# A routed two-layer expert stage on one core: eight pairs of token tiles in place of three

## The chip, the cores and the metric

One core of a Trainium2 chip runs the whole program once. The metric is device time in microseconds (us); lower is better. The kernel before took a median of 958.46 us in 3 runs (958.34 to 959.61). Engines are named as in the profile: PE (TensorE), DVE (VectorE), ACT (ScalarE), POOL (GpSimd), SP (SyncE, which here only starts DMAs).

## The reference

```python
def reference(...):                      # cut to what matters
    attn = _attn_ref(q, k, v)            # [4, 8, 768, 64] recurrent attention with decay
    x = attn as rows                     # 3072 tokens x 512
    x = (max(h, 0) + alpha * min(h, 0)) @ w_out      where h = x @ w_in       # 512 -> 2048 -> 512
    logits = cosine(x, expert_emb) / tau             # 8 experts
    e = argmax(logits);  gate = softmax(logits)[e]
    out = gate * (max(x @ w1[e], 0) @ w2[e])         # 512 -> 1024 -> 512, one expert per token
```

Only the last line is the subject here: each token goes through the two matrices of its own expert. The routing depends on the data.

## The kernel before

Tokens come out of the attention and of the first two-layer stage in six chunks of 512. The router ranks the tokens of each chunk, and POOL scatters each row into a table in HBM that holds one region of `CAP` rows for each expert. The expert stage, from about 614 us on, walks that table in **tiles of 128 rows**. All matrix products are taken in three passes (high x high, low x high, high x low), so every operand is split into a high part (ACT, a cast) and a low part (DVE, a subtraction).

The weights of one expert are 4 MB, loaded as four **chunks** of 1 MB: chunks 0 and 1 are w1, chunks 2 and 3 are w2. A chunk goes from HBM into its own staging buffer `raw[m]` (there is one of each, four in all), ACT casts it into the weight buffer `W` (`split_expert` on ACT, L1516), DVE subtracts (`split_expert` on DVE, L1233). `W` has two slots that alternate. Each loading of an expert's weights is a **run**, numbered from 0. SP's `expert_weights(e, run)` issues the four loads in the order 0, 1, 2, 3; each waits until DVE has split the same chunk of the run before (`s_lo`), and since SP works in order, a later load waits for the earlier ones too.

The stage has two parts. First **three pairs**: two tiles of the same expert are taken together. `up_two(i, g)` (L841, four groups of 24 matmuls with 256 columns) makes the hidden values already transposed; `h_two_high` (ACT) and `h_two_low` (DVE) split them; `expert_down(t, ...)` (L879) makes the output of each tile. `x_transpose(i, tt)` (L711) turns the rows of a later tile (`tt` steps after tile `4 * i`) in the middle of an `expert_down`. The three pairs are chosen (`choose_pairs`) from the counts of the first five chunks of tokens, from whole groups of 256 rows, so that they can start before the last chunk is ranked.

Then **single tiles**, from tile `LEAD` = 6 on, in the order of the experts (`perm`: the fullest one first, then the others by number). A single tile is `up` (L819, 24 matmuls of 512 columns), `x_transpose` of the tile two further on, and `expert_down` with `h_transpose` (L856) of the next tile in its middle. Every expert gets at least one single tile (`ntile` is raised to 1). `T_NEXT` holds, for a tile that begins an expert, the number of the next expert. ACT's `tile(t)` does, in this order: `w1_part` (casts w1 chunks of the expert after that of tile t+1, if tile t+1 begins one), `relu_half(t+1)`, `x_hi_part(t+2)`, `load_rows` (of tile t+3), `w2_part` (casts w2 chunks of the expert after that of tile t), `h_hi_part(t+1)`, `y_part(t)`. DVE's `tile(t)` has the same parts in the same order, with `relu_half` ahead of `w1_part`. The engines run in order, so what stands behind a cast that waits for a chunk waits as well.

`pads` writes 128 rows of padding behind each expert's last row, eight DMAs from SP. `load_rows` brings 128 rows of the table; in the pairs it is issued from SP, in the single tiles from ACT's queue. POOL scatters each finished tile to `out` (L1739).

## Time and profile before

| | us |
|---|---|
| median of 3 runs | 958.46 |
| profiled execution, its own time | 958.03 |
| span of the profiled execution | 955.7 |
| around the span (958.03 - 955.7) | 2.3 |
| PE busy | 944.6 (99%) |
| DVE busy | 605.5 (63%) |
| ACT busy | 274.2 (29%) |
| POOL busy | 250.2 (26%) |
| granted TensorE clock, mean | 0.997 |

A row of the timeline gives the start, the duration, engine, source line, operation, output<-input, count, and in brackets how long the engine had been idle and what ended that. Instructions of one kind that follow each other are merged into one row. The landing time of a DMA is counted from its issue.

### The profile page before, as it was taken

The numbers are of one execution on the slowest core, as the hardware profiler recorded it, in microseconds if no ns is written. First come the engines' busy times: TensorE is split into PE (matmuls) and PEld (weight loads), VectorE is DVE, ScalarE is ACT, GpSimd is POOL, SyncE is SP. The second block draws the span as 40 slices with busy tenths as digits, with TensorE's granted clock in tenths as the row PEclk, the third lists the DMA queues.
The fourth block names the chain that finished last, engine by engine and source line by source line (L and its number), as shares of the span: only waits on it lengthen the run. The fifth ranks groups of instructions, "written<-read, shape, count | busy, mean of one in ns | idle before, by whom it ended". The sixth has DMA issues, their size and how long they took to land.

```text
span 955.7 us, 16603 instructions
## 1 busy us (share of the span) xinstructions
PE 944.6 (99%) x5542; PEld 795.1 (83%) x5543; DVE 605.5 (63%) x1111; ACT 274.2 (29%) x410; POOL 250.2 (26%) x192
## 2 busy tenths in 40 slices
PE   8999999999999999999999999999999999999996
PEld 7888888888888888888888888899888888888885
DVE  5555589647973698459865887787763742523541
ACT  4222121112111211112111222255655543423541
POOL 4443214241424143413432122441100100000001
PEclk9999999999999999999999999999999999999998
DMA  8431297023001400140002302187936461423311
GB/s 307 159 133 56 82 391 235 1 89 133 0 0 45 174 0 0 44 154 1 1 23 78 112 0 88 54 332 271 394 139 255 159 269 44 157 93 119 135 42 54
DMA packets 29142, 115.22 MB, mean 121 GB/s; under 512 B 4864, under 2 KB 5248, under 8 KB 22929
## 3 DMA queue, kind: packets, MB, share of 16 engines
q1 hardware_dynamic: 21584, 96.12, 27.6%
q0 software_dynamic: 4336, 12.61, 3.4%
q10 hardware_dynamic: 3168, 5.79, 2.0%
q8 instruction: 32, 0.52, 0.2%
q14 instruction: 22, 0.17, 0.1%
HBM read 101.88 MB, written 26.30 MB: 134 GB/s over the span
## 4 chain that ended last, share of the span: by engine, by line
PE 98%; DVE 0%; DMA 0%; issue 0%; POOLq 0%; ACT 0%; SPq 0%; DVEq 0%
PE bank L726 28%; PE bank L744 27%; PE bank L879 16%; PE bank L819 12%; PE bank L841 4%; PE bank L621 2%; PE bank L665 2%; PE bank L637 2%; PE bank L856 2%; PE bank L711 1%; PE bank L654 1%; DMA attention<-in_qk 0%; PE bank L690 0%; DVE en_all L970 0%; PE bank L684 0%; PE bank L698 0%
## 5 line engine op out<-in xcount | busy, mean ns | idle before, releaser
L726 PE MATMUL bank<-activations_split,weights_split 128*128 128x512 f32 x1152 | 277.8, 391 | 0.0
L744 PE MATMUL bank<-weights_split,activations_split 128*128 128x512 f32 x1152 | 276.0, 389 | 0.0
L744 PEld LDWEIGHTS bank<-weights_split,activations_split 128*128 128x128 f32 x1152 | 216.2, 188 | 44.8
L726 PEld LDWEIGHTS bank<-activations_split,weights_split 128*128 128x128 f32 x1152 | 215.1, 188 | 45.8 <-issue 1.1
L1681 POOL TENSOR_TENSOR activations_split<-scratch,activations_split 128x512 fp32r<-128x512 f32 x84 | 117.0, 1393 | 311.7 <-ACT activations_split L1436 304.4
L1436 ACT CAST activations_split<-scratch 128x512 fp32r<-128x512 f32 x96 | 59.8, 623 | 412.2 <-DVE scratch L1013 412.2
L879 PE MATMUL bank<-weights_split,activations_split 128*128 (+1 forms) x648 | 159.7, 397 | 0.0
L879 PEld LDWEIGHTS bank<-weights_split,activations_split 128*128 128x128 f32 x648 | 118.1, 188 | 22.6
L1072 DVE SCALAR_TENSOR_TENSOR attention<-rows,en_all 128x512 f32<-128x512 f32 x140 | 135.0, 1005 | 0.5 <-DMA en_all<-en_rows 0.5
L1008 DVE TENSOR_SCALAR scratch<-bank,alpha 128x512 f32<-128x512 f32 x96 | 71.7, 747 | 99.3 <-PE bank L726 98.6
L819 PE MATMUL bank<-weights_split,activations_split 128*128 x504 | 118.2, 390 | 0.1
L819 PEld LDWEIGHTS bank<-weights_split,activations_split 128*128 128x128 f32 x504 | 94.4, 188 | 19.9 <-issue 0.5
L1739 POOL DMA_INDIRECT out<-scratch,y_token x27 | 33.5, 1242 | 277.2 <-ACT scratch L1549 276.9
L1233 DVE TENSOR_TENSOR weights_split<-attention,weights_split 128x2048 f32 (+1 forms) x30 | 67.9, 2285 | 14.1 <-ACT weights_split L1516 13.9
L1226 DVE TENSOR_SCALAR en_all<-bank 128x512 f32<-128x512 f32 x21 | 14.5, 691 | 92.3 <-PE bank L819 92.3
L1013 DVE SCALAR_TENSOR_TENSOR scratch<-bank,scratch 128x512 f32<-128x512 f32 x96 | 66.4, 691 | 3.3
L1516 ACT CAST weights_split<-attention 128x2048 f32 (+1 forms) x30 | 56.7, 1906 | 11.4 <-issue 6.5
L1242 DVE TENSOR_TENSOR activations_split<-bank,activations_split 128x512 fp32r<-128x512 f32 x42 | 26.9, 683 | 25.1 <-ACT activations_split L1535 25.1
L1703 POOL DMA_INDIRECT expert_rows<-rows,slot_i x24 | 31.0, 1290 | 30.0 <-DVE slot_i L1172 25.0
L841 PE MATMUL bank<-activations_split,weights_split 128*128 128x256 f32 x288 | 36.4, 284 | 0.0
L841 PEld LDWEIGHTS bank<-activations_split,weights_split 128*128 128x128 f32 x288 | 35.3, 192 | 0.2
L1535 ACT CAST activations_split<-bank 128x512 fp32r<-128x512 f32 x42 | 22.5, 589 | 38.3 <-PE bank L856 38.3
(216 smaller groups left out, 732.5 us busy)
## 6 DMA issues: line engine op xcount, KB each, us to landing
attention<-in_w_exp SPq DMA_DIRECT2D x33, 1024.0 KB, 6.7
en_all<-in_w_exp SPq DMA_DIRECT2D x11, 1024.0 KB, 6.8
attention<-in_kv SPq DMA_DIRECT2D x43, 256.0 KB, 4.0
expert_rows<-in_pad_rows SPq DMA_DIRECT2D x8, 1285.0 KB, 24.2
rows<-in_w_mlp SPq DMA_DIRECT2D x14, 512.0 KB, 3.5
attention<-in_qk SPq DMA_DIRECT2D x12, 512.0 KB, 5.5
rows<-expert_rows ACTq DMA_DIRECT2D x22, 257.0 KB, 2.7
scratch<-in_qk SPq DMA_DIRECT2D x10, 512.0 KB, 3.8
```

The source lines that it names most:

```text
L726: last = mm(H_ps[f % 2][:, :], win(a, kc, f), x[:, kc, :], start=(k == 0), stop=(k == 3 * KC - 1))
L744: last = mm(bank[j][:, :], x[f % 2][:, j * P:(j + 1) * P], wout(a, f), start=(f == 0 and a == 0 and part_ == "hi"), stop=(f == FB - 1 and ...
L819: last = mm(EH_ps[half][:, :], x[tt % 2][:, kc * P:(kc + 1) * P], W[:, bass.ds(slot * HALF + w1_at(kc, a) + half * 512, 512)], start=(k == ...
L841: last = mm(EH_ps[g % 2][:, j * 2 * P:(j + 1) * 2 * P], W[:, slot + w1_at(kc, a) + fc * P:slot + w1_at(kc, a) + (fc + 1) * P], ex_two[:, b ...
L879: last = mm(EY_ps[tt % 2][:, :], own, W[:, bass.ds(slot * HALF + w2_at(fc, a), DM)], start=(k == 0), stop=(k == 3 * FC - 1))
L1008: ve.tensor_scalar(neg, H_ps[f % 2][:, :], 0.0, alpha_sb[:, f:f + 1], ALU.min, ALU.mult)\
L1013: ve.scalar_tensor_tensor(g_sb[f % 2], H_ps[f % 2][:, :], 0.0, neg, ALU.max, ALU.add)\
L1072: ve.scalar_tensor_tensor(dot_out[n % 2], xrow[j][:, 0:DM], 1.0, EN[:, e * DM:(e + 1) * DM] if e < E - 1 else EN_ps, ALU.mult, ALU.mult, a ...
L1233: ve.tensor_tensor(W[:, bass.ds(at_ + CH, CH)], raw[m], W[:, bass.ds(at_, CH)].bitcast(f32), ALU.subtract).then_inc(s_lo[m // HC], 1)
L1436: se.copy(g_hi[f % 2], g_sb[f % 2]).then_inc(s_gh, 1)
L1516: se.copy(W[:, bass.ds((run % 2) * HALF + raw_at(m), CH)], raw[m]).then_inc(s_hi[m // HC], 1)
L1681: gp.tensor_tensor(g_lo[f % 2], g_sb[f % 2], g_hi[f % 2].bitcast(f32), ALU.subtract)\
```

## The change

The number of pairs goes from 3 to 8 (`PAIRS = E`), so 16 tiles go in pairs and the single tiles begin at `LEAD` = 16. The first three pairs (`EARLY`) are chosen as before. The other five are chosen on DVE from the final counts, in two kinds: first pairs that leave their expert at least one more tile, then the rest; the second tile of such a pair need not be full. Their table entries are ready at `s_late`. Each of the five pairs loads its expert's weights for itself, so there are 16 runs of weights instead of 11. The padding is 256 rows for each expert instead of 128, and `CAP` grows by 128. In the pairs, the w1 chunks of the next run are split during the two `expert_down` of this pair, the w2 chunks during the next pair's `up_two`; in the last pair, w2 of the run after it is split there too, ahead of its w1. Rows for tiles 6 and 7 come from SP behind all four loads of run 3; from tile 8 on ACT issues them.

```diff
@@ -32,7 +32,7 @@
...
     return dict(B=B, H=H, S=S, D=D, DM=DM, F=F, E=E, F2=F2, N=n, NC=S // P, HP=H // 2,
-                CAP=n + P, TILES=n // P + E - 1)
+                CAP=n + 2 * P, TILES=n // P + E - 1)
...
+    EARLY, PAIRS = 3, E
+    LEAD = 2 * PAIRS
+    ALONE = TILES - LEAD
...
-        r = eng.value_load(tab[0:1, bass.ds(T_ROW + t - LEAD, 1)], min_val=0, max_val=PAD)
+        if isinstance(t, int) and t < LEAD:
+            r = eng.value_load(tab[0:1, T_PROW + t // 2:T_PROW + t // 2 + 1], min_val=0, max_val=PAD - 2 * P)
+            r = r + t % 2 * P
+        else:
+            r = eng.value_load(tab[0:1, bass.ds(T_ROW + t - LEAD, 1)], min_val=0, max_val=PAD)
         eng.dma_start(xrow[tt % 4][:, :], table[bass.ds(r, P), :]).then_inc(s_xld[tt % 4], 16)
...
         for e in range(E):
-            r = eng.value_load(tab[0:1, T_PADS + e:T_PADS + e + 1], min_val=0, max_val=PAD - P)
-            eng.dma_start(table[bass.ds(r, P), :], pad_rows[0:P, :]).then_inc(s_pads, 16)
+            r = eng.value_load(tab[0:1, T_PADS + e:T_PADS + e + 1], min_val=0, max_val=PAD - 2 * P)
+            eng.dma_start(table[bass.ds(r, 2 * P), :], pad_rows[0:2 * P, :]).then_inc(s_pads, 16)
...
@@ -589,11 +599,13 @@
             pads(sp)
             sp.wait_ge(s_pad0, due(s_pad0, 16))
             sp.wait_ge(s_pads, due(s_pads, 16 * E))
-            expert_weights(sp.value_load(tab[0:1, T_PERM:T_PERM + 1], min_val=0, max_val=E - 1), PAIRS)
-            sp.wait_ge(s_tab, due(s_tab, 1))
-            load_rows(sp, 1, 2)
-            load_rows(sp, 1, 3)
-            with sp.Fori(PAIRS + 1, PAIRS + E) as run:
+            sp.wait_ge(s_late, due(s_late, 1))
+            for run in range(EARLY, PAIRS):
+                expert_weights(sp.value_load(tab[0:1, T_PEXP + run:T_PEXP + run + 1], min_val=0, max_val=E - 1), run)
+                if run == EARLY:
+                    load_rows(sp, 1, 2)
+                    load_rows(sp, 1, 3)
+            with sp.Fori(PAIRS, PAIRS + E) as run:
                 expert_weights(sp.value_load(tab[0:1, bass.ds(T_PERM - PAIRS + run, 1)], min_val=0, max_val=E - 1), run)
...
+            for i in range(1, PAIRS):
+                for g in range(4):
+                    up_two(i, g)
+                t = 2 * i
+                more = i + 1 < PAIRS
+                expert_down(t, t, None, between=(lambda: x_transpose((t + 2) // 4, (t + 2) % 4)) if more else None)
+                expert_down(t + 1, t + 1, None, between=lambda: x_transpose((t + 2 + more) // 4, (t + 2 + more) % 4))
...
+            e = expert_of(t0)
+            up(t0, 0, 0, e)
+            x_transpose(i0, 1)
+            up(t0, 0, 1, e)
+            e_next = expert_of(t0 + 1)
+            up(t0 + 1, 1, 0, e_next)
+            h_transpose(t0)
+            up(t0 + 1, 1, 1, e_next)
+            x_transpose(i0, 2)
+            expert_down(t0, 0, e, between=lambda: h_transpose(t0 + 1))
...
             h_two_low(0, 3)
             split_expert(1, (0,))
             x_lo_part(2, 2)
-            split_expert(1, (1, 2))
+            split_expert(1, (1,))
+
+            early, kinds, lens, ends, rows, off, places, used_up = (scratch(n) for n in range(8))
+            dve.wait_ge(s_cnt, due(s_cnt, 1))
+            link(ve.tensor_copy(cnt[o, :], CNT_ps[o, :]))
+            ve.scalar_tensor_tensor(tab[o, T_PADS:T_PADS + E], cnt[o, :], float(FILL), base[o, :], ALU.max, ALU.add).then_inc(s_pt, 1)
+            link(ve.tensor_scalar(t_off[o, :], t_end[o, :], float(EARLY), None, ALU.min))
+            link(ve.tensor_copy(early[:, 0:1], t_off[o, 0:1]))
+            link(ve.tensor_tensor(early[:, 1:E], t_off[o, 1:E], t_off[o, 0:E - 1], ALU.subtract))
             x_lo_part(3, 3)
...
+
+            h_two_low(1, 0)
+            split_expert(1, (2,))
+            h_two_low(1, 1)
             split_expert(1, (3,))
...
+            by_place(cnt)
+            link(ve.tensor_tensor(over[o], bc(cnt_at[o, :], NT), const("steps")[o].unsqueeze(1).broadcast_to([1, E, NT]),
+                                  ALU.is_gt))
+            by_kind = C[o, QD:QD + E * NT].rearrange("p (e m s) -> p s e m", e=E, s=2)
+            link(ve.tensor_reduce(kinds[:, 0:E], by_kind[:, 0], AX, ALU.add))
+            link(ve.tensor_reduce(kinds[:, E:2 * E], by_kind[:, 1], AX, ALU.add))
...
+            split_expert(2, (0,))
+            x_lo_part(4, 4)
+            split_expert(2, (1,))
+
+            link(ve.scalar_tensor_tensor(lens[:, 0:E], kinds[:, 0:E], -1.0, early[:, 0:E], ALU.add, ALU.subtract))
...
+            link(ve.tensor_tensor(lens[:, E:2 * E], kinds[:, E:2 * E], early[:, 0:E], ALU.subtract))
...
+            x_lo_part(5, 5)
+            LATE = PAIRS - EARLY
+            link(ve.tensor_tensor(off[:, 0:2 * E - 1], rows[:, 1:2 * E], rows[:, 0:2 * E - 1], ALU.subtract))
...
+            link(ve.tensor_tensor(gone, bc(nth, 2 * E), over_late(ends), ALU.is_ge))
+            link(ve.tensor_tensor(moved, gone, over_late(off), ALU.mult))
+            link(ve.tensor_reduce(row_f[o, 0:LATE], moved, AX, ALU.add))
+            link(ve.scalar_tensor_tensor(row_f[o, 0:LATE], nth, 2.0 * P, row_f[o, 0:LATE], ALU.mult, ALU.add))
+            link(ve.tensor_scalar(tab[o, T_PROW + EARLY:T_PROW + PAIRS], row_f[o, 0:LATE], rows[:, 0:1], None, ALU.add))
...
+            link(ve.tensor_scalar(tab[o, T_PEXP + EARLY:T_PEXP + PAIRS], nx[o, 0:LATE], perm[o, 0:1], None, ALU.add))
+            ve.tensor_scalar(used_up, ends, float(LATE), None, ALU.min).then_inc(s_late, 1)
+            dve.wait_ge(s_late, due(s_late, 1))
+
+            h_two_low(2, 0)
+            split_expert(2, (2,))
+            h_two_low(2, 1)
+            split_expert(2, (3,))
+            h_two_low(2, 2)
...
+            h_two_low(2, 3)
+
+            split_expert(3, (0,))
+            x_lo_part(6, 6)
+            split_expert(3, (1,))
             link(ve.tensor_tensor_scan(t_end[o, :], ones[o, 0:E], ntile[o, :], 0.0, ALU.mult, ALU.add))
...
+            link(ve.scalar_tensor_tensor(nx[o, :], eid[o, 1:ALONE + 1], 1.0, nx[o, :], ALU.add, ALU.mult))
+            ve.tensor_copy(tab[o, T_NEXT:T_NEXT + ALONE], nx[o, :]).then_inc(s_tab, 1)
+            h_two_low(3, 3)
+
+            for i in range(3, PAIRS):
+                if i > 3:
+                    h_two_low(i, 0)
+                    split_expert(i, (2,))
+                    h_two_low(i, 1)
+                    split_expert(i, (3,))
+                    h_two_low(i, 2)
+                    if i == PAIRS - 1:
+                        split_expert(PAIRS, (2,))
+                    h_two_low(i, 3)
+                    if i == PAIRS - 1:
+                        split_expert(PAIRS, (3,))
+                split_expert(i + 1, (0,))
+                if i + 1 < PAIRS:
+                    x_lo_part(2 * i + 2, 2 * i + 2)
+                split_expert(i + 1, (1,))
+                x_lo_part(2 * i + 2 + (i + 1 < PAIRS), 2 * i + 2 + (i + 1 < PAIRS))
             w1_part(next_expert(LEAD))
...
-            x_hi_part(5, 1)
...
+            for i in range(PAIRS):
+                t, more = 2 * i, i + 1 < PAIRS
+                if i:
+                    h_two_high(i, 0)
+                    split_expert(i, (2,))
+                    h_two_high(i, 1)
+                    split_expert(i, (3,))
+                    h_two_high(i, 2)
+                    if not more:
+                        split_expert(PAIRS, (2,))
+                    h_two_high(i, 3)
+                    if not more:
+                        split_expert(PAIRS, (3,))
+                split_expert(i + 1, (0,))
+                if more:
+                    x_hi_part(t + 2, t + 2)
+                split_expert(i + 1, (1,))
+                y_part(t, t // 4, t % 4)
+                if i == 2:
+                    act.wait_ge(s_late, due(s_late, 1))
+                    act.wait_ge(s_pads, due(s_pads, 16 * E))
+                if i == PAIRS - 2:
+                    act.wait_ge(s_tab, due(s_tab, 1))
+                if i >= 2:
+                    load_rows(act, t // 4 + 1, t % 4)
+                x_hi_part(t + 2 + more, t + 2 + more)
+                if not more:
+                    w1_part(next_expert(LEAD), LEAD - 1)
+                y_part(t + 1, t // 4, t % 4 + 1)
+                if 2 <= i and more:
+                    load_rows(act, t // 4 + 1, t % 4 + 1)
+            relu_half(LEAD)
+            x_hi_part(LEAD + 1, 1)
+            h_hi_part(LEAD, 0)
...
+            e = next_expert(LEAD)
+            for tt in range(4):
+                e = tile(LEAD // 4, tt, e)
+            with act.Fori(LEAD // 4 + 1, SURE // 4) as i:
                 e = next_expert(4 * i)
```

## Rows read from the trace of the kernel before

**Rows 1.** The profile page, the chain of work that ended last, by engine.
```profile
PE 98%; DVE 0%; DMA 0%; issue 0%; POOLq 0%; ACT 0%; SPq 0%; DVEq 0%
```
**Rows 2.** Busy time by stretch (columns named in first row): one pair, one single tile.
```profile
core 0: us, PE busy (x) PEld busy (x) DVE busy (x) ACT busy (x) POOL busy (x), PEclk, DMA share, GB/s
644.00:667.38 23.38, 23.38 (x154) 21.31 (x152) 18.78 (x44) 12.30 (x14) 4.36 (x2) 1.00 0.76 269
709.71:721.95 12.24, 12.24 (x62) 10.24 (x61) 8.91 (x8) 7.63 (x11) 1.75 (x1) 1.00 0.78 300
```
**Rows 3.** Timeline of PE in the pair of tiles 2 and 3.
```profile
644.00 11.68 PE L841 MATMUL bank<-activations_split,weights_split 128*128 128x256 f32 x96
...
658.26 0.60 PE L711 MATMUL bank<-constants,rows 128*128 128x128 f32 x4
```
**Rows 4.** Timeline of PE around single tile 11.
```profile
755.09 1.03 PE L856 MATMUL bank<-constants,en_all 128*128 128x128 f32 x8
...
758.69 5.61 PE L819 MATMUL bank<-weights_split,activations_split 128*128 x24
764.14 0.60 PE L711 MATMUL bank<-constants,rows 128*128 128x128 f32 x4
```
**Rows 5.** Groups of instructions on the profile page: the scatters of finished tiles.
```profile
L1739 POOL DMA_INDIRECT out<-scratch,y_token x27 | 33.5, 1242 | 277.2 <-ACT scratch L1549 276.9
```
**Rows 6.** Timeline of SP, the DMA issues of the pairs.
```profile
645.13 0.33 SPq L546 DMA_DIRECT2D en_all<-in_w_exp  x1
647.03 1.44 SPq L588 DMA_DIRECT2D rows<-expert_rows  x2
650.50 9.69 SPq L408 DMA_DIRECT2D expert_rows<-in_pad_rows  x8
663.78 3.06 SPq L546 DMA_DIRECT2D attention<-in_w_exp  x3
...
670.25 1.45 SPq L396 DMA_DIRECT2D rows<-expert_rows  x2
```
**Rows 7.** Timeline of SP, loads of chunks 2 and 3, then chunks 0 and 1.
```profile
760.33 0.33 SPq L546 DMA_DIRECT2D attention<-in_w_exp  x1
762.53 0.33 SPq L546 DMA_DIRECT2D en_all<-in_w_exp  x1
...
764.15 1.00 SPq L546 DMA_DIRECT2D attention<-in_w_exp  x2
```
**Rows 8.** Issues with KB and landing time, of 711.48, 713.68, 764.82, 670.25 us.
```profile
attention<-in_w_exp SPq DMA_DIRECT2D x1, 1024.0 KB, 4.6
...
en_all<-in_w_exp SPq DMA_DIRECT2D x1, 1024.0 KB, 5.6
...
attention<-in_w_exp SPq DMA_DIRECT2D x1, 1024.0 KB, 9.9
...
rows<-expert_rows SPq DMA_DIRECT2D x1, 257.0 KB, 8.9
```
**Rows 9.** Timeline of DVE: a weight split in pair 2, one in single tile 11.
```profile
675.76 2.29 DVE L1233 TENSOR_TENSOR weights_split<-attention,weights_split 128x2048 fp32r<-128x2048 f32 x1
...
760.02 2.29 DVE L1233 TENSOR_TENSOR weights_split<-en_all,weights_split 128x2048 f32 x1
```
**Rows 10.** Timeline of ACT: row cast to weight cast; a weight cast that waited, and relu.
```profile
715.78 0.59 ACT L1505 CAST activations_split<-bank 128x512 fp32r<-128x512 f32 x1 [2.56 <-PE bank L711]
...
717.16 1.90 ACT L1516 CAST weights_split<-attention 128x2048 f32 x1 [0.79 <-issue]
...
751.80 1.91 ACT L1516 CAST weights_split<-attention 128x2048 f32 x1 [1.77 <-DMA attention<-in_w_exp]
...
753.62 0.58 ACT L1511 ACTIVATE en_all<-bank 128x512 f32<-128x512 f32 x1
```
**Rows 11.** Busy time by stretch, during the first filling of the table, HBM to HBM.
```profile
140.00:145.00 5.00, 5.00 (x23) 4.13 (x22) 4.96 (x11) 1.25 (x3) 2.80 (x2) 1.00 1.02 342
```
**Rows 12.** Busy time by stretch, after PE's last matmul (948.0 us).
```profile
950.00:955.70 5.70, 0.00 (x0) 0.00 (x0) 0.00 (x0) 0.00 (x0) 0.58 (x1) 0.58 0.09 35
```

More of the change, by code:

```diff
@@ L323, in build @@
     s_star, s_tail, s_fill = sem("star"), sem("tail"), sem("fill")
-    s_pair, s_tail2 = sem("pair"), sem("tail2")
+    s_pair, s_tail2, s_late = sem("pair"), sem("tail2"), sem("late")
     s_lg = sem("lg")
@@ L905, in _ @@
             expert_down(1, 1, None, between=lambda: x_transpose(0, 3))
[L906 to L926 removed]
+            for i in range(1, PAIRS):
[5 more added lines that the diff above has]
+                expert_down(t + 1, t + 1, None, between=lambda: x_transpose((t + 2 + more) // 4, (t + 2 + more) % 4))
+            i0, t0 = LEAD // 4, LEAD
+            pe.wait_ge(s_tab, due(s_tab, 1))
+            e = expert_of(t0)
[8 more added lines that the diff above has]
+            expert_down(t0, 0, e, between=lambda: h_transpose(t0 + 1))
+            e = e_next
+            for tt in range(1, 4):
+                e = tile(i0, tt, e)
+            with pe.Fori(i0 + 1, SURE // 4) as i:
                 e = expert_of(4 * i)
@@ new lines, in _ @@
+            link(ve.tensor_tensor_scan(ends, ones[o, 0:2 * E], lens, 0.0, ALU.mult, ALU.add))
+            link(ve.tensor_copy(places[:, 0:E], perm[o, :]))
+            link(ve.tensor_copy(places[:, E:2 * E], perm[o, :]))
+            link(ve.tensor_scalar(rows[:, 0:E], perm[o, :], float(CAP), None, ALU.mult))
+            link(ve.scalar_tensor_tensor(rows[:, 0:E], early[:, 0:E], 2.0 * P, rows[:, 0:E], ALU.mult, ALU.add))
+            link(ve.scalar_tensor_tensor(rows[:, E:2 * E], lens[:, 0:E], 2.0 * P, rows[:, 0:E], ALU.mult, ALU.add))
@@ new lines, in _, with over_late @@
+            gone, moved = (C[o, QD + n * 96:QD + n * 96 + LATE * 2 * E].rearrange("p (t e) -> p t e", t=LATE) for n in range(2))
+            def over_late(ap):
+                return ap.unsqueeze(1).broadcast_to([1, LATE, 2 * E])
+            nth = const("tile")[o, 0:LATE]
+            link(ve.tensor_tensor(gone, bc(nth, 2 * E), over_late(ends), ALU.is_ge))
+            link(ve.tensor_tensor(moved, gone, over_late(off), ALU.mult))
+            link(ve.tensor_reduce(row_f[o, 0:LATE], moved, AX, ALU.add))
@@ L1360, in _ @@
[L1360 to L1370 removed]
+            link(ve.scalar_tensor_tensor(row_f[o, :], nth, float(P), row_f[o, :], ALU.mult, ALU.add))
@@ L1387, in _ @@
             e = next_expert(LEAD)
-            for tt in (2, 3):
-                e = tile(1, tt, e)
-            with dve.Fori(2, SURE // 4) as i:
+            for tt in range(4):
+                e = tile(LEAD // 4, tt, e)
+            with dve.Fori(LEAD // 4 + 1, SURE // 4) as i:
                 e = next_expert(4 * i)
@@ L1610, in tile @@
                 return e_next
-            e = tile(1, 2, next_expert(LEAD))
-            e = tile(1, 3, e)
-            with act.Fori(2, SURE // 4) as i:
+            e = next_expert(LEAD)
+            for tt in range(4):
+                e = tile(LEAD // 4, tt, e)
+            with act.Fori(LEAD // 4 + 1, SURE // 4) as i:
                 e = next_expert(4 * i)
```

151 lines of the change are left out of this document (51 added, 100 removed).

## The prediction

> **What bounds the kernel now.** I read the chain of waits first: 98% of the span is PE work [rows 1], with TensorE at full clock. Then the expert stage by stretch: a pair of tiles takes 23.38 us, a single tile 12.24 us, with PE busy throughout in both [rows 2]. Then who is next late. In a single tile that changes expert, DVE is busy 8.91 us and ACT 7.63 us of 12.24, and the DMA engines have a share of 0.78 [rows 2]: that is near the limit, and it happens rarely. Last the order of the loads on SP and of the casts on ACT. Around tile 11, the only place where two tiles in a row begin an expert behind the pairs' hand-over, ACT waited 1.77 us for a chunk and did its relu at 753.62, and PE took the result at 755.09 [rows 4, 10]: under 1 us to spare. A PE-bound kernel gains only what is taken off PE, and loses every wait that reaches it.
>
> **What the change takes off PE.** Five pairs stand in place of ten single tiles: 2 x 12.24 - 23.38 = 1.10 us each [rows 2], so 5.5 us in all. The number of tiles doesn't move. Routing the reference's inputs gives the experts 552, 55, 579, 631, 564, 222, 373 and 96 tokens, that is 5, 1, 5, 5, 5, 2, 3, 1 tiles, 27 in all, as many as the scatters in the trace [rows 5]. In the order of places (expert 3 first) the early pairs are two of place 0 and one of place 1. The five late ones are one of place 1, two of place 3 and two of place 4. Left as single tiles before: 1, 3, 1, 5, 5, 2, 3, 1. After: 1, 1, 1, 1, 1, 2, 3, 1, which is 11, without an empty one.
>
> **The order of the weights in the single tiles: the large term.** Six tiles in a row (16 to 21) now begin an expert. In the iteration of tile t ACT first casts w1 for tile t+2, then does relu of t+1, x of t+2, starts a row load, and then casts w2 for tile t+1. SP issues chunks 0 to 3 of a run in order and each waits for DVE's split of the run before. So chunks 0 and 1 of run r+1 can't be issued until chunk 3 of run r is, and that waits for the last w2 split of an iteration (at X). ACT needs these chunks 0 and 1 at once, ahead of relu. The trace has the four loads behind such an X: DVE ended at 760.02 + 2.29 = 762.31 [rows 9], chunk 3 went out at 762.53, chunks 0 and 1 at 764.15 and 764.82 (the two rows merged, the second starts 0.33 before the end) [rows 7], and the last landed 9.9 us later [rows 8], at 774.7, so 12.4 us after X. Then follow ACT's cast 1.9 and relu 0.6; from the start of x's cast to the start of the next weight cast 717.16 - 715.78 = 1.4; two casts of 1.9 [rows 10]; and DVE's last split 2.3 [rows 9]. That closes the ring: 12.4 + 1.9 + 0.6 + 1.4 + 3.8 + 2.3 = 22.4 us for a tile, where PE needs 12.24. PE stands before `h_transpose(t+1)`, in the middle of `expert_down(t)`. The iterations of tiles 17 to 20 pay it (in that of tile 21 no w1 is due, since tile 22 has the expert of tile 21): about 10 us each. Unrolled from the hand-over below, the first wait comes to 9.8 and the others to 22.4 - 12.24 = 10.1. I take 40 us. Lower bound: if the last chunk landed after 5.6 us as one with little before it does [rows 8], the ring would be 18.1 and the term 23.
>
> By the Trainium skill (DMA: Bandwidth & Descriptors, Anatomy of one DMA) a DMA takes about 2 us and then its bytes at 436 GB/s; its 4.4 us for one chunk agrees with the 4.6 measured alone [rows 8]. For four chunks behind each other it would give 11.6 from the first issue, where the trace has 774.7 - 760.33 = 14.4 [rows 7, 8]; the four waits would be some 11 us less in all, and the total 998. I go by the trace.
>
> **Hand-over from pairs to single tiles.** Let T be the start of the last pair. A second w2 split on DVE ends at T + 10.7 in this pattern (675.76 + 2.29, with the pair at 667.38 [rows 2, 9]), the first one split and one low part earlier, at T + 7.8. Run 8's chunk 2 goes out then, lands 4.6 later [rows 8] and is cast by T + 14.5, with `h_two_high(7, 3)` behind it on ACT and `h_two_low` on DVE behind its split, at T + 17.4. PE wants that at T + 11.5 (`up_two`) + 2.8 (half of the `expert_down`) + 1.0 (four matmuls) = T + 15.3: 2.1 us. Chunk 3 goes out at T + 10.9 and lands after 5.6 [rows 8]; behind it ACT has the casts of chunks 0 and 1, y, a row load, then x of tile 16, to T + 25.2, and DVE's part ends at T + 26.7, where PE would be at T + 23.2. Together 3.5 us. Next, run 9's chunk 1 is free only at T + 26.1, lands at T + 31.6, and cast, split and x of tile 17 end at T + 36.4; PE is there at T + 32.5: 4 us. Nothing in the trace stands in this order, so the bounds are wide: 2 for both together, and 13 if these loads took up to 9.9 as well [rows 8].
>
> **Rows behind weights on SP, in pairs 1 and 2.** Run 1's w2 is now split during `up_two(1)`, not before it. Run 2's chunk 3, issued at 645.13 before [rows 6], goes out at 644.0 + 10.9 = 654.9. Tile 4's rows follow 1.9 behind (647.03 - 645.13 [rows 6]), at 656.8. The chunk lands 5.6 later [rows 8], the rows some 0.5 behind it, at 661.0. PE transposes them at 658.26 [rows 3]: 2.7 us. Bounds 0 and 5.
>
> The eight padding DMAs are issued 1.3 us apart [rows 6] and now move 4.2 MB; at the 342 GB/s of the first filling [rows 11] they take 12.3 us. Begun behind chunk 3, they are down at about 674, and run 3 can start at 674.3, where before it started at 663.78 [rows 6]. From that issue to the landing of tile 6's rows it took 670.25 + 8.9 - 663.78 = 15.4 us with the four loads between [rows 6, 8]: now 689.7. Tile 6 is transposed 14.3 into its pair (644.00 to 658.26 [rows 3]), and that pair starts at 670.1, so PE is there at 684.4: 5.3. If the loads were further apart, as chunk 3's own wait makes them, 2.8. I take 4.5; bounds 1 and 10.
>
> **What costs nothing.** DVE's selection of the late pairs is about 50 steps on one partition; they stand between splits in pairs of which DVE is busy 18.78 of 23.38 us [rows 2], about 10 us over three pairs, and `x_lo_part(5)` keeps under 1 us to spare. `s_late` comes before the pads have landed, so it delays nothing. If that cover went, 2 us. From pair 3 on, the loads of a run have over 20 us. ACT's row loads for tiles 8 and on are a pair ahead. The wait of ACT for the pads stands before a load, x and y of tile 7; the pads are long down there.
>
> **The clock.** After PE's last matmul the granted clock falls: 0.58 over the last 5.7 us [rows 12], so between the full 2.4 GHz and 1.2 GHz. Waits of 10 us will bring it down too. In the ring that costs nothing as long as a tile's PE work fits in 22.4 us. Behind the last wait it costs what runs slowly: between 0 and one tile, 12; I take 2.
>
> **The sum.** -5.5 + 40 + 3.5 + 4 + 2.7 + 4.5 + 2 = +51.2. The profiled execution would have a span of 955.7 + 51.2 = 1006.9 and a time of 1009.2 with the 2.3 around it; its time was 0.4 under the median of the runs. I predict 1009 us.
>
> **Rivals.**
> (a) The ring is shorter than I make it, because chunks land sooner without the other traffic: 18 us for a tile, waits of 23 in all, about 992. For it: chunks took 4.6 to 9.9 us in the same stage [rows 8]. Against: four of them always stand together here.
> (b) PE falls to half clock in every wait and doesn't come back within a tile. 2 x 12.24 = 24.5 exceeds 22.4, so PE sets the pace: 4 x 2.1 more, and up to 12 behind the last wait, about 1027. The Trainium skill describes this pattern (TensorE: Matmul & The Clock Gate, HAM oscillation): each burst behind a DMA wait starts cold. Here only the end of the span shows the clock fall, and no row shows how soon it returns.
> (c) Order doesn't matter, only bytes. A tile with a load moves 4.2 MB and 0.5 MB of rows in and out; at 300 GB/s with a share of 0.78 [rows 2], that is 385 GB/s at full share, 12.3 us, just a tile. Then only the hand-over and row waits stay: about 967. Against it: ACT and SP are in order.
> (d) Faster: the round trip of a chunk (free, loaded, cast, split, free) stays under 12.2 us, so that no wait reaches PE anywhere, and 5.5 are gained: 952.5. It decides at X: this needs chunks 0 and 1 there before ACT asks, and SP issues them only afterwards.
> (e) The change doesn't keep 27 tiles: an expert used up in pairs would still take an empty single tile, 12 to 22 us for each, from 1021 on. Against it stands the way the late pairs are taken.
>
> **How the numbers follow.** The forecast has 0.60, and its own range is 998 to 1020. (a) 0.15, (b) 0.12, (c) 0.08, (d) 0.03, (e) 0.02. The range of 985 to 1028 takes in (a), most of (b), and the bounds of the hand-over and row terms. A measurement of this kernel can tell about 0.2%, 2 us, from no change: faster 0.03, same 0.01, slower 0.96.
>
> **What would show it.** PE waiting for ACT before `h_transpose` of tiles 18 to 21, some 10 us each and 22 us apart; before it, ACT's weight cast waiting for the DMA, with three of SP's loads within 3 us. Shorter waits of PE for rows before `x_transpose` of tiles 4 and 6, and before `up` of tile 17. Pairs 3 to 6 at 23.4 us without a wait. If PE waits nowhere, in-order SP and ACT are not what I take them for; if pairs 3 to 6 wait, the cover in the pairs was mis-read; if tiles 18 to 21 wait much less, the landing times are.

## The result and the profile after

| | before | after |
|---|---|---|
| median, us | 958.40 (958.34 to 959.61, 4 runs) | 1012.66 (1011.13 to 1013.6, 4 runs) |
| ratio after / before | | 1.0561 (95% interval 1.0543 to 1.058) |
| span of the profiled execution, us | 955.7 | 1011.0 |
| granted TensorE clock, mean | 0.997 | 0.975 |
| PE busy, us | 944.6 | 956.5 |

The change makes the kernel 54 us slower. The page's chain of work that ended last, for the kernel after, by engine; it answers to [rows 1]:

```profile
PE 83%; DMA 6%; DVE 4%; ACT 3%; issue 2%; SPq 1%; ACTq 1%; POOLq 0%; DVEq 0%
```

PE held 98% of that chain and now holds 83%. Most of the rest went to DMA, DVE and ACT, which handle a new expert's weights (and, for DMA, the rows). Next, every instruction of PE from 640 us on that had to wait (timeline of PE; line numbers are those of the kernel after and differ a little in the other kernels; here L723 is `x_transpose`, L891 `expert_down`, L831 `up`, L868 `h_transpose`):

```profile
661.12 0.66 PE L723 MATMUL bank<-constants,rows 128*128 128x128 f32 x4 [1.86 <-DMA rows<-expert_rows]
690.21 1.11 PE L723 MATMUL bank<-constants,rows 128*128 128x128 f32 x4 [3.91 <-DMA rows<-expert_rows]
809.66 1.20 PE L891 MATMUL bank<-weights_split,activations_split 128*128 128x512 f32 x4 [0.90 <-ACT activations_split L1652]
812.10 4.84 PE L891 MATMUL bank<-weights_split,activations_split 128*128 128x512 f32 x20 [1.24 <-DVE activations_split L1262]
831.85 5.23 PE L831 MATMUL bank<-weights_split,activations_split 128*128 x12 [5.79 <-DVE activations_split L1233]
865.14 1.97 PE L868 MATMUL bank<-constants,en_all 128*128 128x128 f32 x8 [8.96 <-ACT en_all L1600]
886.42 1.97 PE L868 MATMUL bank<-constants,en_all 128*128 128x128 f32 x8 [6.14 <-ACT en_all L1600]
907.70 1.97 PE L868 MATMUL bank<-constants,en_all 128*128 128x128 f32 x8 [6.49 <-ACT en_all L1600]
930.17 1.97 PE L868 MATMUL bank<-constants,en_all 128*128 128x128 f32 x8 [8.07 <-ACT en_all L1600]
```

Nine waits, in three families: two for the rows of tiles 4 and 6, three at the hand-over from pairs to single tiles, and four before `h_transpose` of tiles 18 to 21, 21.3 to 22.5 us apart. The last four come from one closed chain of waits through SP, ACT and DVE, the ring. One turn of it (timelines of SP, ACT and DVE; L1605 and L1247 the cast and split of weights, L1600 `relu_half`, L556 the loads of weights, `en_all` the staging buffer of chunk 3):

```profile
851.32 0.33 SPq L556 DMA_DIRECT2D en_all<-in_w_exp  x1
852.94 17.57 SPq L556 DMA_DIRECT2D attention<-in_w_exp  x3
872.38 0.33 SPq L556 DMA_DIRECT2D en_all<-in_w_exp  x1
...
860.30 1.90 ACT L1605 CAST weights_split<-attention 128x2048 f32 x1 [10.97 <-DMA attention<-in_w_exp]
862.69 1.90 ACT L1605 CAST weights_split<-attention 128x2048 f32 x1 [0.50 <-DMA attention<-in_w_exp]
864.50 0.59 ACT L1600 ACTIVATE en_all<-bank 128x512 f32<-128x512 f32 x1
...
848.80 2.29 DVE L1247 TENSOR_TENSOR weights_split<-en_all,weights_split 128x2048 f32 x1
862.49 4.57 DVE L1247 TENSOR_TENSOR weights_split<-attention,weights_split 128x2048 f32 x2 [8.79 <-ACT weights_split L1605]
867.66 2.29 DVE L1247 TENSOR_TENSOR weights_split<-attention,weights_split 128x2048 f32 x1
869.87 2.28 DVE L1247 TENSOR_TENSOR weights_split<-en_all,weights_split 128x2048 f32 x1
```

DVE ends the last w2 split at 848.80 + 2.29 = 851.09. Only then does SP issue chunk 3 (851.32) and, behind it, chunks 0 and 1 (from 852.94). ACT sits in front of the cast of chunk 0 for 10.97 us, until 860.30; only after both casts comes the relu that PE is waiting for (864.50). The next such end is 869.87 + 2.28 = 872.15: 21.1 us a turn.

Where the 55.3 us of span (1011.0 - 955.7) are, by stretches of PE's timeline in the two kernels, each beside what it takes without waits (22.92 for pair 7 is what the fastest kernel below takes, from 785.01 to 807.93):

| stretch | us |
|---|---|
| five pairs for ten single tiles, last pair included | -5.7 |
| start of pair 1 (644.84, before 644.00) | +0.8 |
| pair 1, 27.04 against 23.38: 2.0 late for the rows of tile 4, the rest slow clock | +3.7 |
| pair 2, 28.93 against 23.38: 4.1 late for the rows of tile 6, the rest slow clock | +5.5 |
| pair 7, 25.64 against 22.92 | +2.7 |
| from `up(16)` to `up(18)`, 27.39 against 19.22 (in before 690.49 to 709.71) | +8.2 |
| from `up(18)` at 847.37 to `up(22)` at 936.38, 89.01 against 4 x 12.24 = 48.96 | +40.05 |
| sum | 55.2 |

Pairs 3 to 6 took 23.36 to 23.41 us each, with no wait.

### The profile page after: what moved, and what is told of

It is laid out like the page before. It is cut to its first block, busy times and chain, and to the rows that moved or that the text cites. A ratio compares the mean times of both kernels' runs of the same rounds, so it can differ in the third digit from the quotient of the medians.

```text
span 1011.0 us, 16202 instructions
## 1 busy us (share of the span) xinstructions
PE 956.5 (95%) x5702; PEld 810.9 (80%) x5702; DVE 649.2 (64%) x1150; ACT 305.1 (30%) x419; POOL 245.5 (24%) x192
## 4 chain that ended last, share of the span: by engine, by line
PE 83%; DMA 6%; DVE 4%; ACT 3%; issue 2%; SPq 1%; ACTq 1%; POOLq 0%; DVEq 0%
PE bank L738 26%; PE bank L756 26%; PE bank L891 11%; PE bank L853 7%; DMA attention<-in_w_exp 5%; DVE weights_split L1247 3%; PE bank L831 3%; PE bank L633 2%; PE bank L677 2%; ACT weights_split L1605 2%; PE bank L649 2%; PE bank L666 1%; DMA rows<-expert_rows 1%; PE bank L723 1%; PE bank L868 1%
## 5 line engine op out<-in xcount | busy, mean ns | idle before, releaser
L756 PEld LDWEIGHTS bank<-weights_split,activations_split 128*128 128x128 f32 x1152 | 216.1, 188 | 44.8
L738 PEld LDWEIGHTS bank<-activations_split,weights_split 128*128 128x128 f32 x1152 | 215.0, 188 | 45.8 <-issue 1.0
L891 PE MATMUL bank<-weights_split,activations_split 128*128 128x512 f32 (+1 forms) x648 | 167.8, 412 | 2.1 <-DVE activations_split L1262 1.2
L891 PEld LDWEIGHTS bank<-weights_split,activations_split 128*128 128x128 f32 x648 | 125.2, 199 | 28.4 <-DVE activations_split L1262 1.7
L1247 DVE TENSOR_TENSOR weights_split<-attention,weights_split 128x2048 fp32r<-128x2048 f32 (+1 forms) x45 | 102.8, 2292 | 61.7 <-ACT weights_split L1605 61.4
L1605 ACT CAST weights_split<-attention 128x2048 fp32r<-128x2048 f32 (+1 forms) x45 | 85.4, 1904 | 55.4 <-DMA attention<-in_w_exp 52.9
L853 PE MATMUL bank<-activations_split,weights_split 128*128 128x256 f32 x768 | 94.8, 283 | 0.0
L853 PEld LDWEIGHTS bank<-activations_split,weights_split 128*128 128x128 f32 x768 | 93.6, 192 | 0.6
L831 PE MATMUL bank<-weights_split,activations_split 128*128 x264 | 64.6, 401 | 5.8 <-DVE activations_split L1233 5.8
L831 PEld LDWEIGHTS bank<-weights_split,activations_split 128*128 128x128 f32 x264 | 51.0, 194 | 17.0 <-issue 6.2
L1262 DVE SCALAR_TENSOR_TENSOR activations_split<-bank,activations_split 128x512 fp32r<-128x512 f32 x32 | 22.0, 688 | 36.4 <-ACT activations_split L1652 36.2
L868 PE MATMUL bank<-constants,en_all 128*128 128x128 f32 x88 | 15.1, 328 | 29.7 <-ACT en_all L1600 29.7
L868 PEld LDWEIGHTS bank<-constants,en_all 128*128 128x128 f32 x88 | 12.8, 170 | 32.3 <-ACT en_all L1600 31.5
```

Source lines behind the costliest of these rows:

```text
L738: last = mm(H_ps[f % 2][:, :], win(a, kc, f), x[:, kc, :], start=(k == 0), stop=(k == 3 * KC - 1))
L756: last = mm(bank[j][:, :], x[f % 2][:, j * P:(j + 1) * P], wout(a, f), start=(f == 0 and a == 0 and part_ == "hi"), stop=(f == FB - 1 and ...
L831: last = mm(EH_ps[half][:, :], x[tt % 2][:, kc * P:(kc + 1) * P], W[:, bass.ds(slot * HALF + w1_at(kc, a) + half * 512, 512)], start=(k == ...
L853: last = mm(EH_ps[g % 2][:, j * 2 * P:(j + 1) * 2 * P], W[:, slot + w1_at(kc, a) + fc * P:slot + w1_at(kc, a) + (fc + 1) * P], ex_two[:, b ...
L891: last = mm(EY_ps[tt % 2][:, :], own, W[:, bass.ds(slot * HALF + w2_at(fc, a), DM)], start=(k == 0), stop=(k == 3 * FC - 1))
L1247: ve.tensor_tensor(W[:, bass.ds(at_ + CH, CH)], raw[m], W[:, bass.ds(at_, CH)].bitcast(f32), ALU.subtract).then_inc(s_lo[m // HC], 1)
```

## The experiments

The theory: SP issues chunks 0 to 3 of a run in order, so that chunk 0 and 1 of the next run, whose staging buffers are long free, go out only behind chunk 3; this closes a ring of 21 to 22 us. The rivals: the bytes of a new expert for each tile; ACT's order, in which the cast that waits stands ahead of relu; the number of tiles that begin an expert being a cost that any order would pay.

**SP's order alone.**

```diff
-            with sp.Fori(PAIRS, PAIRS + E) as run:
-                expert_weights(..., run)                       # chunks 0, 1, 2, 3 of each run
+            order = list(((0, 0), (0, 1), (0, 2), (0, 3), (1, 2), (1, 3), (1, 0), (1, 1), (2, 0), (2, 1)))
+            for n in range(3, E):
+                order += [(n, 0), (n, 1), (n - 1, 2), (n - 1, 3)]
+            order += [(E - 1, 2), (E - 1, 3)]
```

> The changed kernel (1012.7 us), with one thing different: for the single tiles SP issues the chunks in the order in which they come free and are wanted (w1 of run r+1 ahead of w2 of run r), not run by run. The same 16 runs, the same bytes, the same order on ACT, DVE and PE. Theory 1 (the ring closes through SP's order): chunks 0 and 1 go out some 7 us earlier and no longer behind X, so the waits of PE before h_transpose of tiles 18 to 21 shrink from 6 to 9 us to under 1, and with them goes the slow clock behind the last: 1012.7 - 40 = about 973, range 968 to 980. The waits before x_transpose of tiles 4 and 6, in the last pair and before up(17) stay. Theory 2 (bytes: 4 MB of weights and 0.5 MB of rows a tile can't be moved faster): the waits stay, about 1010. Theory 3 (ACT's order alone makes the waits, since relu stands behind the w1 casts): they stay at 5 us or more each, over 990.

Measured: 975.81 us (973.05 to 976.8, 4 runs), ratio to before 1.0178 (1.0159 to 1.0197), so 36.9 us less than after. The four waits became one. The timeline of PE in this kernel from 833 us on holds a single wait, and its window over two of these single tiles shows why bytes are not the limit:

```profile
870.61 1.09 PE L878 MATMUL bank<-constants,en_all 128*128 128x128 f32 x8 [0.95 <-ACT en_all L1610]
...
core 0: us, PE busy (x) PEld busy (x) DVE busy (x) ACT busy (x) POOL busy (x), PEclk, DMA share, GB/s
875.00:899.50 24.50, 24.50 (x121) 20.43 (x120) 22.31 (x17) 19.27 (x21) 2.29 (x2) 1.00 0.96 363
```

The same bytes, the same casts in the same order on ACT, the same number of new experts, and PE is busy 24.50 of 24.50 us. The ring ran through SP's order. The DMA share of 0.96 says that bytes are not far behind.

**The order on ACT and DVE** (SP as in after). The lines shown are ACT's; on DVE `w1_part` moves behind `x_lo_part(t + 2)` in the same way.

```diff
                 e_next = next_expert(t + 1)
-                w1_part(e_next, t)
                 relu_half(t + 1)
...
                 load_rows(act, i, tt + 3)
+                w1_part(e_next, t)
                 w2_part(e, t)
```

> The changed kernel, with one thing different: in the loop of single tiles ACT and DVE take w1 of the expert after next behind relu, x and (on ACT) the row load, not ahead of them. SP's order stays. Theory 1 (the ring closes through SP's order): the ring keeps nearly its length, since the last w2 split still stands behind the w1 chunks, and PE waits as long at another place, before up(t+2) for the low part of w1, instead of before h_transpose: 8 to 10 us each, total 1000 to 1013. Theory 3 (ACT's order alone): relu comes at once and the waits go, about 973. Theory 2 (bytes): about 1010, as in theory 1, so this run tells 3 from the other two.

Measured: 1012.22 us (one run). PE no longer waits before `h_transpose`, but, one step on, before `up` of the next tile, for DVE's split of w1, and at the end once before `expert_down`:

```profile
849.84 7.36 PE L831 MATMUL bank<-weights_split,activations_split 128*128 x24 [1.87 <-DVE weights_split L1247]
871.21 7.61 PE L831 MATMUL bank<-weights_split,activations_split 128*128 x24 [7.20 <-DVE weights_split L1247]
892.59 7.18 PE L831 MATMUL bank<-weights_split,activations_split 128*128 x24 [6.98 <-DVE weights_split L1247]
914.28 8.21 PE L831 MATMUL bank<-weights_split,activations_split 128*128 x24 [7.71 <-DVE weights_split L1247]
939.72 4.61 PE L891 MATMUL bank<-weights_split,activations_split 128*128 x12 [4.54 <-DVE weights_split L1247]
```

The first four stand 21.4 to 21.7 us apart, and the five come to 28.3 us, where the four of after are 29.7. Relu is where the wait was seen, not what made it.

**A quarter of each chunk.** In the single tiles from the third one's run on, only a quarter of each chunk is loaded; the rest of the computation is unchanged, on partly old weights.

> The changed kernel, with the order of everything kept, but from the third run of the single tiles on only a quarter of each chunk is loaded (1/4 of 1 MB; casts and splits work on the whole chunk, so the results of those experts are not the reference's). Theory 1: the ring keeps its order and its ACT and DVE work, but the last chunk lands some 5.5 us behind X instead of 12.4: ring 22.3 - 7 = about 15.4, waits of PE of 2 to 4 us instead of 6 to 9, four times -7 = -28: about 985, range 978 to 992. Theory 2 (bytes alone): no wait is left, 1012.7 - 40 = 973 or less. Theory 3 (ACT's own work and order alone, whatever the loads do): no change, 1010 or more.

Measured: 993.34 us (one run), 1.3 us above the expected range. The ring turns in 16.4 to 16.6 us, where 15.4 was expected, and the waits stay, at 1.3 to 4.0 us. Timelines of DVE, SP and ACT in this kernel:

```profile
852.25 2.29 DVE L1252 TENSOR_TENSOR weights_split<-en_all,weights_split 128x2048 f32 x1
...
855.81 13.94 SPq L613 DMA_DIRECT2D attention<-in_w_exp  x3
...
859.42 1.90 ACT L1610 CAST weights_split<-attention 128x2048 f32 x1 [6.65 <-DMA attention<-in_w_exp]
```

From the end of the split (854.54) to the cast of chunk 0 it takes 4.9 us where after has 860.30 - 851.09 = 9.2. The three quarters of the bytes that are gone were about 5 us of a turn. What stays, some 16.5 us, is the last quarter, issue, landing, casts and splits one behind the other, and is over 12.24 by itself. The expectation had put the cast of chunk 1 at 5.5 us behind the split; it starts at 861.23, 6.7 behind it, because chunk 0's cast is in its way, and that is the 1 us that the turn is longer.

**Six pairs.** `PAIRS = 6`, with the tables sized for it.

> The changed kernel with six pairs instead of eight (12 tiles in pairs, 15 single tiles 1, 1, 1, 1, 5, 2, 3, 1; 14 runs of weights). Theory 1: one ring iteration fewer (three waits of PE before h_transpose, of tiles 14 to 16, not four), so -10, and two pairs fewer, +2.2: 1012.7 - 8 = about 1005, range 1001 to 1009. Each of the other waits stays. Theory 2 (bytes): two runs fewer are 8.4 MB, at 385 GB/s 22 us: about 991. That the number of pairs as such costs (something in pairs 3 to 7): 1012.7 times nothing in the ring but 2/5 of 54, about 991 too.

Measured: 1003.7 us (one run), three ring waits of 9.53, 6.38 and 6.72 us: one tile less that begins an expert takes one turn's excess away. The theory said 1005, the one by bytes 991.

**Rows ahead of the weights in pairs 1 and 2.**

```diff
-            expert_weights(..., 2)
+            expert_weights(e2, 2, (0, 1))
             ...                                    # rows of tiles 4 and 5, pads
+            expert_weights(..., 2, (2, 3))
...
+                expert_weights(e_run, run, (0, 1))
                 if run == EARLY:
                     load_rows(sp, 1, 2)
                     load_rows(sp, 1, 3)
+                expert_weights(e_run, run, (2, 3))
```

> The changed kernel, with SP's order in the pairs changed: rows of tiles 4 and 5 and the eight pads go out behind chunk 1 of run 2, ahead of its chunks 2 and 3; rows of tiles 6 and 7 behind chunk 1 of run 3. Nothing else. If the waits before x_transpose of tiles 4 and 6 (2.0 and 4.1 us in the changed kernel) come from the place behind the weights and the pads, as predicted, both go, and with each the slow clock behind it (1.6 and 1.5 us more than the same work takes at full clock): 1012.7 - 9.2 = about 1003.5, range 1001 to 1006. If they come from the selection of the late pairs or from DMA traffic, they stay and nothing moves.

Measured: 1001.43 us (one run), 11.2 less than after. Neither `x_transpose(4)` nor `x_transpose(6)` waits; the first wait of PE behind 640 us is the one at 799.81.

**Padding of 128 rows again.**

```diff
-            eng.dma_start(table[bass.ds(r, 2 * P), :], pad_rows[0:2 * P, :]).then_inc(s_pads, 16)
+            eng.dma_start(table[bass.ds(r, P), :], pad_rows[0:P, :]).then_inc(s_pads, 16)
```

> The changed kernel with 128 rows of padding for each expert instead of 256 (no tile of these counts reads further). The pads then move 2.1 MB, are bound by their issue at 1.3 us each and land some 3 to 5 us sooner. If the padding delays run 3 and so the rows of tile 6 behind it, as predicted, the wait before x_transpose(6) shrinks from 4 to 5 us to about 2.5 (the floor that chunk 3's own wait sets), total 1012.7 - 2 = about 1010.7, range 1009 to 1012. If the pads don't matter, 1012.7.

Measured: 1011.57 us (one run), 1.1 less than after and within the spread of after's runs. The wait before `x_transpose(6)` is 3.93 us, where about 2.5 was expected and after has 3.91. SP's timelines, first after, then this kernel:

```profile
659.12 9.69 SPq L418 DMA_DIRECT2D expert_rows<-in_pad_rows  x8
676.93 3.25 SPq L556 DMA_DIRECT2D attention<-in_w_exp  x3
```

```profile
659.29 9.68 SPq L418 DMA_DIRECT2D expert_rows<-in_pad_rows  x8
673.82 5.06 SPq L556 DMA_DIRECT2D attention<-in_w_exp  x3
```

Run 3's loads start 3.1 us sooner with half the padding, but its chunk 3, which tile 6's rows stand behind, only 683.07 - 681.76 = 1.3 sooner. Even that is not the padding: chunk 3 waits for DVE and goes out 11.19 us behind the start of pair 2 in both kernels (671.88 and 670.57), and pair 2 began 1.3 sooner here because the clock stayed up behind the wait for tile 4's rows. In five other kernels with the large padding and the same order of rows (those with SP's order alone, ACT's and DVE's order, six pairs, busy PE and quarter chunks) the wait before `x_transpose(6)` is 4.90 to 5.28 us. So the size of the padding is worth between nothing and 1.4 us of that wait, and these runs don't say more. The order costs more than the size.

**PE kept busy in the waits**, with 12 small matmuls before `up(17)` and 18 before each of the four `h_transpose`; nothing else changes.

> The changed kernel with idle matmuls on PE into a free bank in the long waits: 18 (about 7.5 us) before h_transpose of tiles 18 to 21, 12 (about 5 us) before up(17). They shorten no wait of the ring, they only keep PE at work. Theory: slow clock costs nothing inside the ring and costs 2.7 us behind its last wait and 2.3 behind the wait at tile 17 (read from the changed kernel's trace): 1012.7 - 5 = about 1007.7, range 1005 to 1010, the ring still 21 to 22 us long. If the slow clock also lengthens the ring (PE's part of a tile is in it), the ring shortens too and the total falls under 1003. If the clock costs nothing, 1012.7.

Measured: 1008.93 us (one run), 3.7 less than after. The rows behind the waits, in after (that of `up(17)`, 831.85, stands above) and then in this kernel:

```profile
930.17 1.97 PE L868 MATMUL bank<-constants,en_all 128*128 128x128 f32 x8 [8.07 <-ACT en_all L1600]
931.78 4.76 PE L891 MATMUL bank<-weights_split,activations_split 128*128 x12
```

```profile
832.78 3.01 PE L831 MATMUL bank<-weights_split,activations_split 128*128 x12 [2.96 <-DVE activations_split L1238]
928.70 1.09 PE L868 MATMUL bank<-constants,en_all 128*128 128x128 f32 x8 [1.89 <-ACT en_all L1605]
929.55 2.99 PE L895 MATMUL bank<-weights_split,activations_split 128*128 x12
```

The first 12 matmuls behind the wait take 3.01 us where after had 5.23, and behind the last ring wait 2.99 where it had 4.76. The turns of the ring stay at 21.0 to 21.2: more work of PE inside them costs nothing, and a faster PE gains nothing there.

**All orders together, then the last wait.** The first kernel has SP's order of rows ahead of weights in the pairs, and w2 of run 8 rounded and split behind x of tile 17 in place of ahead of w1. For the single tiles it has SP's order of the first experiment with one difference, which follows from that move: w1 of runs 9 and 10 goes out ahead of w2 of run 9, and not behind it. The second kernel moves chunk 0 of run 8 (cast on ACT, split on DVE) forward into the last `up_two`:

```diff
                     h_two_high(i, 2)
+                    if not more:
+                        split_expert(PAIRS, (0,))
                     h_two_high(i, 3)
-                split_expert(i + 1, (0,))
+                if more:
+                    split_expert(i + 1, (0,))
```

> The changed kernel with SP's order of e1 (chunks as they come free), SP's order of e4 in the pairs, and at the hand-over w2 of run 8 no longer split inside the last pair but behind x of tile 17 (on ACT and DVE). All waits of PE but one of 2 to 3 us before up(17) should be gone: 958.4 - 5.5 (five pairs) + 2.5 (that wait) + 1 to 2 (the slow clock behind it) + 0 to 1 (waits under 0.5 in the single tiles) = about 957.5, range 954 to 962. If the theory of the waits is incomplete, it stays over 965.

> Eight pairs with the issue order of e8_all, and the first chunk of w1 of run 8 rounded and split (ACT and DVE) already behind the third group of up_two of the last pair, the second chunk behind the last group, so that the loads of w1 of run 9 are issued two to three us sooner. If the only wait left in e8_all (2.2 us before up(17), and the 1.7 us of slower clock behind it) is set by that chain, both go: 957.07 - 3.9 = 953.2 us (952 to 956), ratio to before about 0.9945, and TensorE runs at full clock through the first single tiles. If the wait is set by something else (the bytes in flight at the change from pairs to single tiles), the time stays at 957.

> The same orders with six pairs in place of eight. Theory that with the waits gone the pairs give what their stages show (1.10 us a pair less work of TensorE): two pairs fewer cost 2.2 us, so 2.2 above e9_best, about 955.4 (954 to 958). Theory that the single tiles are bound by the bytes of a new expert each: two of them fewer, so it would be as fast as e9_best or faster.

| | median, us | ratio to before |
|---|---|---|
| all orders, eight pairs | 957.07 (955.52 to 959.19, 10 runs) | 0.9985 (0.9975 to 0.9994) |
| chunk 0 forward too, eight pairs | 953.76 (953.3 to 955.45, 5 runs) | 0.9953 (0.9939 to 0.9966) |
| the same with six pairs | 956.19 (955.7 to 958.07, 11 runs) | 0.9977 (0.9968 to 0.9986) |

The first came out as expected, 957.07 for 957.5, with one wait of PE behind 640 us, before `up(17)`:

```profile
816.34 4.54 PE L845 MATMUL bank<-weights_split,activations_split 128*128 x12 [2.23 <-DVE activations_split L1247]
```

In the second this wait is 0.52 us and the 12 matmuls behind it take 3.00, so it was set by the chain of chunk 0, as expected; the kernel is 0.5% faster than before. Windows over its single tiles that begin an expert, and its two waits of PE behind 640 us:

```profile
core 0: us, PE busy (x) PEld busy (x) DVE busy (x) ACT busy (x) POOL busy (x), PEclk, DMA share, GB/s
838.50:850.74 12.24, 12.24 (x62) 10.17 (x61) 11.64 (x9) 10.34 (x11) 0.99 (x1) 1.00 0.99 387
850.74:862.98 12.24, 12.24 (x62) 10.21 (x61) 11.24 (x9) 10.25 (x10) 1.11 (x1) 1.00 0.96 360
...
814.52 3.00 PE L845 MATMUL bank<-weights_split,activations_split 128*128 x12 [0.52 <-DVE activations_split L1247]
873.86 1.09 PE L882 MATMUL bank<-constants,en_all 128*128 128x128 f32 x8 [0.32 <-ACT en_all L1614]
```

PE waits for nothing in these tiles, but it is close: DVE is busy 11.6 of 12.24 us and the DMA engines have a share of 0.99. Two pairs fewer cost 956.19 - 953.76 = 2.4 us, where 2 x 1.10 = 2.2 was expected: with the waits gone, the pairs give what [rows 2] promise, and having two tiles fewer that begin an expert gains nothing.

## Why the prediction was right, point by point

It said 1009 us (985 to 1028), and slower; 1012.66 was measured. The mechanism and the places of all waits were those it named. That the total is so near is in part luck: the clock cost 6.1 us more and `up(17)` 1.8 more than predicted, and the ring, the last pair and the row terms together 4.5 less. The sizes of its terms:

| term | predicted | measured |
|---|---|---|
| five pairs | -5.5 | -5.7 |
| ring of tiles 18 to 21 | +40 | +37.4 |
| last pair | +3.5 | +2.7 |
| `up(17)` | +4 | +5.8 |
| rows of tile 4 | +2.7 | +2.0 |
| rows of tile 6 | +4.5 | +4.1 |
| slow clock | +2 | +8.1 |
| start of pair 1 | 0 | +0.8 |
| sum | +51.2 | +55.2 |

- **The ring.** A turn was worked out as 22.4 us from [rows 7 to 10] and measured as 21.3, 21.3 and 22.5 between the waits. The turn shown above, 872.15 - 851.09 = 21.1, is 1.3 shorter than worked out. Of that, 0.8 is the landing: chunk 1 was there 862.69 - 851.09 = 11.6 us behind DVE's split, not 12.4. The rest is the sequence behind it, 872.15 - 862.69 = 9.5 and not 10.0. Chunk 2 had gone out at 849.11, so four chunks were under way, and from that issue to chunk 1's cast it took 862.69 - 849.11 = 13.6 us. By the formula of the Trainium skill (DMA: Bandwidth & Descriptors, Anatomy of one DMA) four would be an estimated 11.6. The section gives it for DMAs issued on the gpsimd path, which the prediction left out; the loads here go out from SP. It is 2 us too short for these loads behind each other, as it was in the trace of before.
- **The last pair.** Two waits of 0.90 and 1.24 us came where 2.1 was worked out. The second part of that term, x of tile 16, cost nothing; that step was wrong. So PE stood before `up(17)` 0.8 us sooner than the prediction had it, and x of tile 17 was 1.1 us later than that: hence 5.8 there and not 4.
- **Rows of tile 6.** The size is right, but not by the main reading. The padding let run 3 go at 676.93, where 674.3 + 0.8 was worked out, but from that issue to the rows' landing it took 690.2 - 676.9 = 13.3 us and not 15.4, and PE was there at 686.3, later than the 684.4 of the prediction. The run with half the padding shows that the rows go out by chunk 3's own wait for DVE, the other reading that the prediction named. And 4.1 is this run's value: in five other kernels the wait is about 1 us longer.
- **The clock, the term that was mis-sized.** I charged a slow clock behind the last ring wait alone, 2 us. It cost 2.65 there, and another 1.5 to 2.3 behind each of three waits for which I charged nothing: those for the rows of tiles 4 and 6 and the one before `up(17)`. Windows of after behind the row waits and `up(17)`, and around the ring's waits:

```profile
661.00:669.00 8.00, 7.88 (x31) 6.43 (x32) 4.75 (x13) 3.16 (x4) 0.98 (x1) 0.79 1.03 364
690.21:698.00 7.79, 7.79 (x33) 6.47 (x33) 4.38 (x9) 3.16 (x4) 0.98 (x1) 0.80 0.42 142
831.80:835.00 3.20, 3.15 (x8) 2.48 (x9) 0.22 (x1) 0.00 (x0) 0.00 (x0) 0.50 0.97 349
865.00:870.00 5.00, 4.86 (x16) 4.19 (x17) 5.00 (x4) 5.00 (x6) 0.00 (x0) 0.50 0.08 30
872.00:880.00 8.00, 8.00 (x39) 6.52 (x37) 2.05 (x4) 0.35 (x1) 0.98 (x1) 1.00 0.98 359
```

  It is 1.6 and 1.5 us behind the row waits, 2.3 behind the wait before `up(17)`, and 2.65 behind the last ring wait: 8.1 in all. The run with a busy PE took back 2.2 before `up(18)` and, with 4.76 + 1.97 against 2.99 + 1.09, the 2.65 behind the last ring wait; of these 4.9 us, 1.1 went to a longer wait for the rows of tile 6 in that run (5.02 us).
- **Rival (b)** was half right. Every burst behind a ring wait starts at a low clock: the eight transposes behind it take 1.97 us each time and 1.04 elsewhere, and the window from 865 us has a granted clock of 0.50 (1.2 GHz). The Trainium skill describes this (TensorE: Matmul & The Clock Gate, HAM oscillation), and the trace agrees. But at 872 us it is back at 1.00 (2.4 GHz), so a tile takes PE 21.3 - 6.1 = 15.2 us and not 24.5, and fits in the turn. PE did not set the pace. The slow clock shows only as ring waits of 6.1 to 8.1 us in place of 9 to 10.
- **Rivals (a), (c), (d), (e).** The ring was not 18 us. Bytes alone (c) fell with the run that has SP's order changed, though its arithmetic was close: the DMA share is 0.96 there and up to 0.99 in the fastest kernel, so a tile's bytes just fit in a tile. The mechanism of (d) was named rightly, chunks 0 and 1 issued before ACT asks; it needed another order of loads and, at the hand-over, of splits, and then came to within 2 us of its 952.5. There are 27 tiles, as said.
- **The start of pair 1.** It is at 644.84 in after, at 644.74 in the fastest kernel, and at 644.15 in the one with SP's order alone, which has the same code up to there as after; so part of it at least is scatter between runs; the kernels with after's order of loads up to there have 644.15 to 645.23. What the rest is stays open.

## What to carry to other kernels

When loads are issued in order from one engine, each staging buffer's real free time is that of the latest-freed buffer ahead of it: write down for one turn which split frees which load, and compare the closed ring with the time of a tile, before making tiles that need new data stand next to each other. Here the same tiles in the same order on PE cost 1012.66 us with one order of loads and splits and 953.76 with another; SP's order in the single tiles alone brought 36.9 of the 58.9. A wait that is seen behind an engine's cast can be moved by reordering that engine and leave the time as it was (1012.22); look for what makes the ring, not for where it is seen.
